# Token routing between the first two ups, the edge channel mirrored in two parts, a step 3 group in the down banks, and a reordered exit

## What is computed

```python
def reference(x, ...):                                # x: (4, 3072, 256), float32
    X = np.fft.fft(np.fft.fft(x, axis=1), axis=2).real
    # channel mix of each token with the token before it
    prev = shift(X, 1)                                # along the sequence, zero first
    xk, xr = mu_k * X + (1 - mu_k) * prev, mu_r * X + (1 - mu_r) * prev
    k = np.maximum(xk @ w_k, 0)                       # 256 -> 1024
    x = sigmoid(xr @ w_r) * (k * k @ w_v)             # 1024 -> 256
    x = x.reshape(12288, 256)
    # experts: the first 384 tokens of each of the 8 experts, in token order
    logits = x @ w_gate;  e = argmax(logits);  g = softmax(logits)[e]
    # token i has place counts[e]; kept if counts[e] < 384
    y = relu(disp[e] @ w1[e]) @ w2[e]                 # 256 -> 1024 -> 256
    return where(kept, g * y[e, place], 0)
```

## Time and profile before

| | |
|---|---|
| Median of 3 runs | 643.03 us (641.93 to 643.16) |
| Profiled execution | 641.74 us, span 639.9 us |
| TensorE (PE) busy | 618.6 us, 97% of the span |
| VectorE (DVE) busy | 452.6 us, 71% |
| ScalarE (ACT) busy | 320.2 us, 50% |
| GpSimd (POOL) busy | 108.6 us, 17% |
| Chain that ended last | PE 88%, DVE 5%, ACT 3% |

### The profile page before, as it was taken

How to read it: one execution, slowest core, us unless ns; L and a number is a source line. 1 busy time by engine, 2 the same in 40 slices (tenths; PEclk the granted TensorE clock), 3 DMA queues, 4 the chain that set the end, 5 groups by cost and what they waited for, 6 DMA issues and landing times.

```text
span 639.9 us, 10620 instructions
## 1 busy us (share of the span) xinstructions
PE 618.6 (97%) x3470; PEld 530.1 (83%) x3470; DVE 452.6 (71%) x1018; ACT 320.2 (50%) x673; POOL 108.6 (17%) x105
## 2 busy tenths in 40 slices
PE   8989999999999999999999999999994999999996
PEld 5958888888888878887888888788783999999995
DVE  4468678977776588779887766687863777666671
ACT  1566445454536654645444545654542566555550
POOL 0530112020202011202020202020206011111111
PEclk9999999999999999999999999999996999999999
DMA  8947154341410033000000000060005545555000
GB/s 318 284 118 263 61 172 158 109 149 59 166 50 21 1 96 120 16 2 8 2 9 0 8 1 2 2 200 1 4 1 189 182 160 182 182 182 182 25 25 25
DMA packets 39597, 59.70 MB, mean 93 GB/s; under 512 B 4198, under 2 KB 31159, under 8 KB 39548
## 3 DMA queue, kind: packets, MB, share of 16 engines
q1 hardware_dynamic: 35708, 52.59, 24.9%
q0 software_dynamic: 3840, 6.52, 2.9%
HBM read 36.63 MB, written 26.91 MB: 99 GB/s over the span
## 4 chain that ended last, share of the span: by engine, by line
PE 88%; DVE 5%; ACT 3%; issue 2%; DMA 1%; POOL 0%; POOLq 0%; DVEq 0%; ACTq 0%
PE bank L291 66%; PE bank L1045 4%; PE bank L1075 4%; PE bank L991 3%; PE bank L978 3%; PE bank L1003 2%; PE bank L348 2%; PE bank L1078 2%; ACT xt L569 1%; PE bank L1360 1%; DVE square L851 1%; DVE xk_raw L753 1%; ACT xk L603 1%; ACT xt L559 1%; DVE xt L742 1%
## 5 line engine op out<-in xcount | busy, mean ns | idle before, releaser
L291 PE MATMUL bank<-k,wv 128*128 128x512 f32 x672 | 166.5, 398 | 0.0
L291 PEld LDWEIGHTS bank<-k,wv 128*128 128x128 f32 x672 | 125.7, 188 | 29.7
L291 PE MATMUL bank<-xk,wk 128*128 128x512 f32 x522 | 132.9, 401 | 0.0
L620 ACT ACTIVATE relu<-bank 128x512 f32<-128x512 f32 x116 | 67.7, 597 | 123.8 <-PE bank L291 70.6
L506 POOL DMA_INDIRECT dispatched<-rows,slot x56 | 64.1, 1144 | 382.8 <-DVE slot L834 370.0
L291 PEld LDWEIGHTS bank<-xk,wk 128*128 128x128 f32 x522 | 96.0, 188 | 21.1
L851 DVE TENSOR_TENSOR square<-relu 128x512 f32<-128x512 f32 x116 | 78.9, 691 | 47.5 <-ACT relu L620 37.4
L846 DVE TENSOR_TENSOR k<-square,k 128x512 fp32r<-128x512 f32 x115 | 79.0, 687 | 4.8 <-ACT k L615 4.8
L615 ACT ACTIVATE k<-square 128x512 fp32r<-128x512 f32 x115 | 72.0, 626 | 13.0 <-DVE square L851 13.0
L291 PE MATMUL bank<-down_w,he 128*128 128x256 f32 x576 | 70.9, 284 | 0.0
L291 PEld LDWEIGHTS bank<-down_w,he 128*128 128x128 f32 x576 | 69.6, 192 | 0.0
(11 more groups left out here) (115 smaller groups left out, 791.5 us busy)
## 6 DMA issues: line engine op xcount, KB each, us to landing
out_rows<-blank SPq DMA_DIRECT2D x16, 768.0 KB
raw_up<-in_moe_w SPq DMA_DIRECT2D x8, 1024.0 KB, 4.7
raw_down<-in_moe_w SPq DMA_DIRECT2D x8, 1024.0 KB
x_area<-in_x SPq DMA_DIRECT2D x12, 512.0 KB, 3.8
dispatched<-blank SPq DMA_DIRECT2D x1, 3276.0 KB, 19.3
got<-dispatched SPq DMA_DIRECT2D x8, 409.5 KB, 6.6
y<-in_x SPq DMA_DIRECT2D x6, 512.0 KB
first_partner<-in_x SPq DMA_DIRECT2D x2, 512.0 KB
```

The lines of the kernel that those rows point to most:

```text
L291: done = nc.tensor.matmul(bank, w, x, start=first and i == 0, stop=last and i == len(terms) - 1)
L620: nc.scalar.activation(relu[:, f % 2, :], hb[f % 2][:, :], ACT.Relu).then_inc(hb_drained, 1)
```

## The change

- In tiles that are not the first of a batch, TensorE runs up 0, the rows, up 1, then one half of the first gate product, the counts, and the rest. ScalarE and VectorE put routing ahead of block 1 accordingly.
- `route_place` keeps the next slot and a limit for each expert instead of adding the expert's base in a step of its own: six steps up to the slots, where there were seven. `base` is still kept for the flag of full experts.
- Step 3 group 1 of later batches uses the down banks `vb`; down 0 waits for its sums.
- After step 3 only the first 4 of 24 rows of the edge channel are mirrored before the next tile's first differences; the other 20 follow in that tile, between ScalarE's blocks 5 and 6.
- SP itself waits for all scatters; `all_routed` is gone. TensorE runs four warm-up matmuls behind the last tile, ahead of the end of the block, and none after the first turn.
- The first product of each expert takes high and low parts as they become ready. `gates` comes behind the expert's hidden blocks, and the release of expert 0's weights ahead of `turned(0, 0)`.

```diff
-    ROUTE_STEPS = 15
+    ROUTE_STEPS = 14
-    first_pairs, later_pairs = [(hb[0], hb[1]), (rb[0], rb[1])], [(rb[0], rb[1])]
+    h_pair, v_pair, r_pair = (hb[0], hb[1]), (vb[0], vb[1]), (rb[0], rb[1])
+    first_pairs, later_pairs = [h_pair, r_pair], [r_pair]
+    first_quads, later_quads = [h_pair, r_pair, h_pair, r_pair], [r_pair, v_pair, r_pair, r_pair]
...
# SP: exit
-                sp.wait_ge(all_routed, 1)
+                sp.wait_ge(scattered, sp.snap(sent, min_val=16 * GRP, max_val=16 * GRP * NTILE))
...
# GpSimd
-                    pool.wait_ge(slots_ready, m + 1)
                     pool.wait_ge(row_copied, CREDIT + GRP * (m + 1))
+                    pool.wait_ge(slots_ready, m + 1)
...
-                pool.wait_ge(scattered, pool.snap(sent, min_val=16 * GRP, max_val=16 * GRP * NTILE))
-                pool.sem_inc(all_routed, 1)
...
# ScalarE
                     hidden(n, 0)
-                    hidden(n, 1)
+                    if n % TILES == 0:
+                        hidden(n, 1)
                     if n > 0:
                         route(n - 1)
+                    if n % TILES:
+                        hidden(n, 1)
...
                     hidden(n, 5)
+                    if n > 0 and n % TILES == 0:
+                        slot0(0, TOK // N1, N2)
+                        slot0(1, TOK // N1, N2).then_inc(slot0_all, 1)
...
                         mirrors(seq, 3)
+                        act.wait_ge(s3_mirrored, DH * QUADS * (seq + 1))
+                        slot0(0, 0, TOK // N1).then_inc(slot0_near, 1)
                     if seq == 1 and PAIRING <= n <= STEP3:
                         up0_part(n - PAIRING)
                     hidden(n, 7)
...
                     elif stage == STEP3:
-                        act.wait_ge(s3_mirrored, DH * QUADS * (seq + 1))
-                        slot0(0, 0, N2)
                         act.wait_ge(edge_in, 16 * (seq + 1))
-                        slot0(1, 0, N2).then_inc(slot0_all, 1)
+                        slot0(1, 0, TOK // N1).then_inc(slot0_near, 1)
...
# VectorE
+                    nc.vector.tensor_scalar(next_slot[:, :], expert_no, float(cap), None, ALU.mult)
+                    nc.vector.tensor_scalar(limit[:, :], expert_no, float(cap), float(cap), ALU.mult, ALU.add)
...
-                                                 base[:, :].unsqueeze(1).to_broadcast(wide), ALU.add))
-                    step(nc.vector.tensor_scalar(over[:, :, :], pos[:, :, :], float(cap), FAR, ALU.is_ge, ALU.mult))
-                    step(nc.vector.tensor_tensor(over[:, :, :], over[:, :, :], pos[:, :, :], ALU.add))
-                    step(nc.vector.scalar_tensor_tensor(pos[:, :, :], expert_no.unsqueeze(1).to_broadcast(wide), float(cap),
-                                                        over[:, :, :], ALU.mult, ALU.add))
+                                                 next_slot[:, :].unsqueeze(1).to_broadcast(wide), ALU.add))
+                    step(nc.vector.tensor_tensor(over[:, :, :], pos[:, :, :], limit[:, :].unsqueeze(1).to_broadcast(wide), ALU.is_ge))
+                    step(nc.vector.scalar_tensor_tensor(pos[:, :, :], over[:, :, :], FAR, pos[:, :, :], ALU.mult, ALU.add))
...
+                    nc.vector.tensor_tensor(next_slot[:, :], next_slot[:, :], total, ALU.add)
...
-                        dve.wait_ge(slot0_all, seq + 1)
+                        dve.wait_ge(slot0_near, DH * seq + 1)
                         difference(0, 0, n + 1)
                         mix(0, 0, n + 1)
+                        dve.wait_ge(slot0_near, DH * (seq + 1))
                         difference(0, 1, n + 1)
...
# TensorE
-                    if g >= len(pairs):
-                        pe.wait_ge(s3_summed, DH * (QUADS * seq + g - len(pairs) + 1))
+                    for user in range(g):
+                        if quads[user] is quads[g]:
+                            pe.wait_ge(s3_summed, DH * (QUADS * seq + user + 1))
...
-                    first_ups(n)
-                    if n > 0:
+                    if n % TILES == 0:
+                        first_ups(n)
+                        if n > 0:
+                            route_rows(n - 1)
+                    else:
+                        pe.wait_ge(mixed, len(MIXED) * n + DH + 1)
+                        up(n, 0)
                         route_rows(n - 1)
+                        up(n, 1)
                     pe.wait_ge(mixed, len(MIXED) * (n + 1) + 1)
                     pe.wait_ge(gated, DH * (n + 1))
-                    gate_in(n, 0)
-                    gate_in(n, 1)
-                    if n > 0:
+                    gate_in(n, 0, 0)
+                    if n % TILES:
+                        route_counts(n - 1)
+                    gate_in(n, 0, 1)
+                    for part in range(DH):
+                        gate_in(n, 1, part)
+                    if n % TILES == 0 and n > 0:
                         route_counts(n - 1)
...
                     elif stage == STEP3:
-                        step3(seq, later_pairs, 1)
+                        pe.wait_ge(row_copied, CREDIT + GRP * n)
+                        step3(seq, later_quads, 1)
...
+                        pe.wait_ge(s3_summed, DH * (QUADS * seq + later_quads.index(v_pair) + 1))
                     down(n, 0)
...
+                walk(pe, before, after, last)
+                keep_warm_with(4, ident, small[:, 0:3 * P])
...
# phase 2, VectorE: gates(e, i) moved from ahead of the loop over f to behind it
# phase 2, TensorE
+                def first_product(e, i):
+                    bank, hidden = hbe[0][:, 0:cap], slice(0, P)
+                    high, low = (w[:, :, hidden] for w in up_w[i])
+                    for h in range(DH):
+                        pe.wait_ge(xe_high, e * DH + h + 1)
+                        nc.tensor.matmul(bank, high[:, h], xe[:, i, 0, h, :], start=h == 0, stop=False)
+                        nc.tensor.matmul(bank, low[:, h], xe[:, i, 0, h, :], start=False, stop=False)
+                    for h in range(DH):
+                        pe.wait_ge(xe_ready, e * DH + h + 1)
+                        done = nc.tensor.matmul(bank, high[:, h], xe[:, i, 1, h, :], start=False, stop=h == DH - 1)
+                    done.then_inc(he_full, 1)
...
-                keep_warm_with(2, ident, small[:, 0:3 * P])
...
-                        pe.wait_ge(xe_ready, (e + 1) * DH)
+                            if f == 0:
+                                first_product(e, i)
+                                continue
```

More of the change, by code:

```diff
@@ L184, in build @@
     base = ph("base", [P, EXPERTS])
+    next_slot = ph("next_slot", [P, EXPERTS])
+    limit = ph("limit", [P, EXPERTS])
     token = ph("token", [P, GRP])
@@ L311, in s2_banks, with s3_banks @@
         return odd[0:ROWS2, 0:(hi - lo) * ZO], even[0:ROWS2, 0:(hi - lo) * ZO]
[L313 to L315 removed]
+    def s3_banks(quads, g):
+        odd, even = quads[g]
         width = QUAD * SCOLS + (N2 if g == 0 else 0)
@@ L432, in _ @@
                 sp.reg_mov(loads, 32)
+                sent = sp.alloc_register("sent_sp")
+                sp.reg_mov(sent, 0)
                 load_weights()
@@ L459, in after @@
                         place_edge(n // TILES + 1)
-                walk(sp, before, after, lambda: None)
+                walk(sp, before, after, lambda: sp.reg_add(sent, sent, 16 * GRP))
                 for c in range(len(CHUNKS)):
@@ L733, in even_out, with sums @@
                                             z[:, lo:hi, P:P + 1].to_broadcast([ROWS2, hi - lo, P // 2]), ALU.add).then_inc(ze_ready, 1)
-                def sums(seq, pairs, g):
-                    even = s3_banks(pairs, g)[1]
+                def sums(seq, quads, g):
+                    even = s3_banks(quads, g)[1]
                     dve.wait_ge(s3_even_full, QUADS * seq + g + 1)
@@ L772, in first_dft @@
                     for g in range(QUADS):
-                        sums(0, first_pairs, g)
+                        sums(0, first_quads, g)
                     dve.wait_ge(consts_in, 16 * CONSTS)
@@ L875, in before @@
                     squares(n, 0)
-                    squares(n, 1)
+                    if n % TILES == 0:
+                        squares(n, 1)
                     if n > 0:
                         route(n - 1)
+                    if n % TILES:
+                        squares(n, 1)
                     squares(n, 2)
                     if stage == STEP3:
-                        sums(seq, later_pairs, 0)
+                        sums(seq, later_quads, 0)
                     squares(n, 3)
@@ L891, in after @@
                     elif stage == STEP3:
-                        sums(seq, later_pairs, 1)
+                        sums(seq, later_quads, 1)
                     squares(n, 5)
@@ L900, in after @@
                     elif stage == STEP3:
-                        sums(seq, later_pairs, 2)
+                        sums(seq, later_quads, 2)
                     early = t < TILES - 1
```

(16 more changed lines are left out.)

42 lines of the change are left out of this document (21 added, 21 removed).

## The result

The changed kernel takes 635.28 us (635.12 to 635.90, 4 runs) beside 642.64 us of the kernel before in the same comparison: ratio 0.9888, 95% interval 0.9871 to 0.9905. A second set of four runs gave 635.84 us (634.31 to 638.02). The profiled execution took 635.90 us, 5.8 less than the profiled one of before; the medians lie 7.4 apart. The forecast was 635.4.

The account below looks back on a forecast made before the run. TensorE, busy for 97% of the span, was taken as the bound, so only the other 3% could gain. Terms 0.7 - 1.1 - 2.0 - 2.3 - 2.9 = -7.6 led to 635.4 us against the median 643.03; range 634.0 to 639.6.

Parts of the forecast that it names:

- Ordinary tiles: Tiles 1 to 5, 7 to 11, 13, 14: work moves, none goes; +0.7 us for 12 tiles.
- the wait of 0.13: In each ordinary tile, TensorE waits 0.13 us at the counts for the one-hot, where it waited 0.07.
- Rival (c): Row copies pile up behind the last row matmul, one-hot 0.93 us later in each of 12 tiles: 647.5 us; chance 0.05.
- Batch changes: Step 3 tiles lose their wait for sums, -1.1 us; tiles 6 and 12 behind them gain 2.0 us.
- the group: Step 3 group 1 in the down banks: group 2 no longer waits for its sums, -1.1 us for two tiles.
- the mirror: Edge channel mirrored only in part before tiles 6 and 12: VectorE starts earlier, gated rows' wait shrinks, -2.0 us.
- Rival (b): At batch changes the mirror's second part delays relu 7 and the next relu 6, nothing gained: 638.5 us; chance 0.12.
- Exit: From the last tile to the turn: earlier counts, one placement step fewer and SP's own wait give -2.3 us.
- scatters, landing and load keep their times: At the exit, scatters keep their time, as do landing (3.00 us) and load (3.00 us).
- about 3.1 behind the fourth scatter's start: Sign at the exit: when the load of the rows would be issued, in us.
- First expert: Start of phase 2: clock stays at 2.4 GHz, next turn 9.85 us after the turn instead of 12.76; -2.9 us.
- rival (a): After the exit the clock falls anyway, next turn 11.35 us behind, gain only 1.4: total 637.1 us; chance 0.28.

Follow-up runs that it names:

- fill_gap: Changed kernel with three more warm-up matmuls at the start of phase 2, in the gap before the turn: 636.15 us.
- route_back: Changed kernel with rows and counts behind both ups and the whole gate product again in every tile: 637.25 us.
- hop_back: Changed kernel with GpSimd waiting for the scatters and signalling SP, as before: 634.53 us.
- warm_back: Changed kernel with the warm-ups in their old place, two behind the first turn and none ahead of the block's end: 637.72 us.
- warm_none: Changed kernel without any warm-up matmul after the tiles: 636.41 us.
- after_again: The changed kernel measured once more with no edit: 635.84 us.
- fill_two_three_2: Changed kernel with two warm-ups ahead of the block's end and three behind it, second set, run for a trace: 636.95 us.
- mirror_whole: Changed kernel with the edge channel mirrored whole ahead of the next tile again: 638.51 us.
- group_back: Changed kernel with all four groups of step 3 using one pair of banks again: 636.77 us.
- after: The changed kernel's first measurement and profile: 635.28 us, profiled execution 635.90 us.

## Why the prediction was right

**Ordinary tiles**, forecast +0.7: +0.3. The one-hot is ready 5.20 behind the tile's start (470.44 + 0.19, forecast 5.19), and the counts start at 5.37, right behind their gate matmuls (470.10 + 3 x 0.235 = 470.81), so the wait of 0.13 is not there: the hand-over passes while the gate matmuls run. What was lost is nearly all in tile 3, where the rows had to wait for x3 behind the addition of the pairing, one of the two that the prediction named as thinnest; the other, tile 9, lost 0.05 (timeline of the changed kernel):

```profile
122.07 0.42 DVE L722 TENSOR_TENSOR x_area<-x_area,y 128x256 f32<-128x256 f32 x1
...
122.40 1.28 DVE L873 TENSOR_TENSOR x<-gate_r,bank 128x512 f32<-128x512 f32 x2
...
123.73 2.12 PE L1058 MATMUL bank<-fan,x 128*128 128x136 f32 x16
```

x3 is done at 123.68, the rows' first matmul starts at 123.73 and the group takes 2.12 instead of 2.02. Rival (c), copies that pile up, is refuted by the 1.73 us in which they follow the banks.

**Batch changes**, forecast -3.1: -3.1. From tile 5's rows to tile 6's it is 36.86 instead of 37.05, and as only tile 5's rows now stand 1.40 earlier in their tile, TensorE gained 1.59. In the same way 36.54 became 36.72, a gain of 1.22, and the step behind tile 12 shrank from 27.68 to 25.98 + 1.40 = 27.38. Undone one at a time, the group costs 1.1 (forecast 1.1) and the mirror 2.0 (forecast 2.0). The cover for the mirror's second part held: the tiles 6 and 12 are not longer behind their rows than before. Rival (b) falls.

**Exit**, forecast -2.3: -1.5. The counts, the placement and GpSimd's start came as worked out (-2.24 together). The step that failed is "scatters, landing and load keep their times". From the first scatter to the load's issue it took 6.85 instead of 7.42: the scatters 0.17 more, but the fourth one's landing 2.32 instead of 3.06, and so the sign "about 3.1 behind the fourth scatter's start" did not come in this trace. The load then took 4.37 to the turn instead of 3.04. Together that is +0.76, nearly all of the 0.8 by which the exit is short of the forecast. Part of the late landing is on SP's side already, for its two load instructions together take 1.28 instead of 0.81 (timelines, before and after):

```profile
485.83 0.81 SPq L412 DMA_DIRECT2D got<-dispatched  x2
...
480.14 1.28 SPq L415 DMA_DIRECT2D got<-dispatched  x2
```

The late landing shows in all profiles in which the load was issued within 3 us of TensorE's last matmul of the tiles (2.6 to 2.9): 3.7 to 4.6 from issue to turn in nine traces, the changed kernel twice and seven variants; in the tenth, fill_gap, the turn stood behind filler. It does not show in the three in which that was over 5 us ago (3.04, 3.15, 3.20; both traces of before and route_back). SP's two instructions divide the traces in the same way: 0.81 in each of the three, 1.22 to 1.89 in all others. It is not SP's wait (hop_back: 4.27) and not the warm-ups (warm_back: 4.34, warm_none: 3.76). Near the moment of leaving ScalarE loads its table, and packets of the instruction queues arrive: between the load's issue and the turn the DMA view counts one or two of them in each of the nine and none in the three. No run took either away, so the cause stays open.

**First expert**, forecast -2.9 with the clock full, -1.4 with rival (a): both were seen. With the full clock the next turn comes 9.69 to 9.77 us behind the turn (after_again, hop_back, fill_gap, fill_two_three_2), against 9.85 forecast. In the first profile and in those of mirror_whole, group_back and route_back it is 11.16, 11.15, 10.78 and 11.76. (The forecast's 9.85 and 11.35 were counted in the chain, which has 9.89 and 11.32 for the two profiles of the changed kernel.) So of the six traces that have both the four warm-ups ahead of the end and the split product, four came out as rival (a) says and two as the forecast, and in these two the clock had been low before. Two runs of the first set, of 635.37 and 635.12 us, have a mean clock of 0.999 and so can't have lost it for long; without a trace, no more is known of them. I had given rival (a) too little. Yet it went wrong in its reason. TensorE's first warm-up came 1.73 us behind its last matmul, so its exit takes nearly as long as ScalarE's 2.08, and TensorE does not use the time of its last matmuls for it, as rival (a) assumed. The Trainium skill's sentence on the deep queue of TensorE (TensorE: Matmul & The Clock Gate, Architectural detail: the array is 16× 32×32, not 1× 128×128) may hold in the tiles; for the leap out of them, the time that I had drawn from it does not. The clock fell behind warm-ups of 2.85 us and a gap of 2.4 us, or else in the hole itself. The prediction had asked only for the gap before the turn, and took 2.9 us from one trace for the time after which the clock falls; in after_again, fill_gap and warm_none it fell 2.2 us behind the last matmul of the tiles, in hop_back 2.3. In route_back it was down before the turn, at about 485.6, 2.4 us behind the last warm-up.

**The sum.** -7.6 was forecast, -7.4 is the difference of the first medians, and 7.0 that of the second set's median to the kernel before beside it (642.83). The tiles gave 0.5 more than the sum, the exit 0.8 less. In the first profile the clock took another 1.4, so its own difference is -5.8. That 635.28 is so near 635.4 is more than the reasons deserve: two terms were off by half a microsecond or more, with opposite signs. Three figures beside the forecast do not follow from its own terms: (a) gives 635.4 + 1.5 = 636.9 and not 637.1, (b) with (a)'s clock 640.0 and not 639.6, and the low end 634.2 and not 634.0. The argument does not hang on them.

## What to carry to other kernels

Where one engine is busy without gaps, add up its stretches and spend effort only in the holes: moving work inside a full tile gained nothing, though it shortened the latency of what hung on it, and this paid once, at the exit. A change in a tail should be judged by differences between milestones in several traces; here the time before the first tile and the clock behind the exit move a run by more than each part is worth. Here a clock that falls in a short pause was not held reliably by one burst of filler ahead of it, and filler placed where it may run at half the clock can push the work that it is for.

## What was not expected of the hardware

- The start: the first tile's rows begin at 68.6 to 70.2 us in the traces of the changed kernel and its variants with the rows moved, though nothing differs there. In the trace of fill_two_three_2 the first matmuls of the transform already start at 9.37, where those of the changed kernel's two traces start at 7.9. This alone moves a run by 1.3 us.
- The clock at the exit: in traces of one and the same kernel it was low from 479.5 to 482.9 (after_again) or from 486.4 to 489.8 (after). Before its fall TensorE had paused from the end of the tiles in the one, and had run warm-ups, paused 2.4 us and begun the turn in the other.
- Leaving the tiles costs 1.7 to 2.1 us on TensorE and 1.9 to 2.2 us on ScalarE, each read as idle time without a releaser ahead of the next instruction.
